# A layer norm's tail tile split ahead of its second pair, and the scaling of q spread over four gates

## The reference, cut to what matters

```python
# attention with a linear kernel, 8 batches, 8 heads, 576 tokens, head size 64
q_s = exp(q - max(q, -1));  q_s = q_s / (sum(q_s, -1) + 1e-9)
k_s = exp(k - max(k, 2));   k_s = k_s / (sum(k_s, 2) + 1e-9)
x = q_s @ (k_s^T @ v)                       # heads side by side: (8, 576, 512)

# first feed-forward block
h = gelu(x @ w_in)                          # w_in 512 x 1024
u, v = h[..., :512], h[..., 512:]
v_n = (v - mean(v)) / sqrt(var(v) + 1e-6) * g_ln
v_s = w_sg @ v_n + b_sg                     # over the 576 tokens
x = x + (u * v_s) @ w_out

# second feed-forward block
h = relu(x @ w_in2);  gate = sigmoid(conv3(h))
out = (h * gate) @ w_out2
```

## Time and profile before

| | |
|---|---|
| median of 3 runs | 922.87 us (921.62 to 923.33) |
| the profiled execution's own time | 924.54 us |
| its span in the trace | 922.6 us |
| PE busy | 905.7 us (98%) |
| DVE busy | 644.9 us (70%) |
| ACT busy | 398.5 us (43%) |
| POOL busy | 371.9 us (40%) |
| granted clock of PE | 0.998 |

### The profile page before, as it was taken

The page is one execution under the profiler, slowest core; times in us unless marked ns, Lnnn a source line. Parts: engine busy times, 40 slices in busy tenths (PEclk is TensorE's granted clock), DMA queues, the critical chain, the costliest instruction groups (busy, mean ns, idle before and its releaser), DMA issues.

```text
span 922.6 us, 14586 instructions
## 1 busy us (share of the span) xinstructions
PE 905.7 (98%) x5852; PEld 843.8 (91%) x5852; DVE 644.9 (70%) x952; ACT 398.5 (43%) x593; POOL 371.9 (40%) x232
## 2 busy tenths in 40 slices
PE   6999999999999999999999999999999999999998
PEld 5799899998998999989989999999999999998987
DVE  6787958678588686765874897866665666757550
ACT  6653544445435444444254254533443343434331
POOL 5773565354472663544514133332232313232320
PEclk9999999999999999999999999999999999999999
DMA  8726674663746546535320302020202020200001
GB/s 294 224 74 230 190 167 154 182 196 123 183 146 175 128 160 179 148 99 137 142 99 30 126 1 87 3 85 23 75 24 86 21 77 23 75 23 24 23 29 52
DMA packets 60034, 99.55 MB, mean 108 GB/s; under 512 B 6720, under 2 KB 25408, under 8 KB 58304
## 3 DMA queue, kind: packets, MB, share of 16 engines
q1 hardware_dynamic: 55360, 89.20, 32.8%
q10 hardware_dynamic: 4608, 9.44, 2.7%
HBM read 78.46 MB, written 19.11 MB: 106 GB/s over the span
## 4 chain that ended last, share of the span: by engine, by line
PE 79%; DVE 6%; POOL 6%; issue 4%; DMA 3%; ACT 2%; SPq 0%; POOLq 0%; DVEq 0%
PE psum L542 45%; PE psum L534 29%; DMA split_arena<-q_rec_dram 2%; DVE plain_arena L1486 2%; PE psum L619 2%; POOL plain_arena L1804 1%; POOL plain_arena L1854 1%; DVE plain_arena L1455 1%; PE psum L655 1%; PE psum L705 1%; POOL split_arena L1848 1%; POOL plain_arena L1811 1%; DMA plain_arena<-in_q_first 1%; PE psum L580 1%; POOL plain_arena L1793 1%
## 5 line engine op out<-in xcount | busy, mean ns | idle before, releaser
L542 PE MATMUL psum<-split_arena 128*128 128x288 f32 x4032 | 558.6, 297 | 1.4 <-DVE split_arena L1518 0.6
L542 PEld LDWEIGHTS psum<-split_arena 128*128 128x128 f32 x4032 | 544.8, 189 | 8.4 <-DVE split_arena L1518 1.9
L534 PE MATMUL psum<-split_arena 128*128 128x512 f32 x1248 | 296.4, 391 | 0.2 <-DVE split_arena L1441 0.2
L534 PEld LDWEIGHTS psum<-split_arena 128*128 128x128 f32 x1248 | 229.9, 188 | 49.3 <-DVE plain_arena L1532 4.3
L1932 POOL TENSOR_TENSOR plain_arena<-plain_arena 128x576 f32<-128x576 f32 x64 | 107.8, 1684 | 277.8 <-ACT plain_arena L1070 277.8
L1577 DVE SCALAR_TENSOR_TENSOR plain_arena<-plain_arena 128x576 f32<-128x576 f32 x64 | 96.2, 1503 | 2.3
L1572 DVE TENSOR_SCALAR plain_arena<-plain_arena 128x576 f32<-128x576 f32 x64 | 36.0, 563 | 87.2 <-ACT plain_arena L1064 87.2
L1064 ACT ACTIVATE plain_arena<-psum 128x576 f32<-128x576 f32 x64 | 41.6, 650 | 105.3 <-PE psum L542 73.9
L1854 POOL TENSOR_TENSOR plain_arena<-plain_arena 128x576 f32<-128x576 f32 x32 | 52.7, 1648 | 62.0 <-DVE plain_arena L1511 62.0
L1843 POOL TENSOR_TENSOR plain_arena<-plain_arena 128x2 f32<-128x2 f32 (+1 forms) x24 | 19.8, 827 | 119.4 <-DVE plain_arena L1472 119.4
L1070 ACT ACTIVATE plain_arena<-plain_arena 128x576 f32<-128x576 f32 x64 | 43.7, 682 | 42.6 <-DVE split_arena L1738 39.5
(11 more groups left out here) (107 smaller groups left out, 831.0 us busy)
## 6 DMA issues: line engine op xcount, KB each, us to landing
x_dram<-plain_arena ACTq DMA_DIRECT2D x32, 288.0 KB, 2.1
plain_arena<-x_dram SPq DMA_DIRECT2D x8, 1152.0 KB, 6.2
out_rows<-plain_arena SPq DMA_DIRECT2D x36, 256.0 KB, 2.0
plain_arena<-in_kT SPq DMA_DIRECT2D x7, 1152.0 KB, 5.4
plain_arena<-in_k SPq DMA_DIRECT2D x7, 1024.0 KB, 5.8
plain_arena<-in_v SPq DMA_DIRECT2D x28, 256.0 KB, 3.9
plain_arena<-in_q_heads SPq DMA_DIRECT2D x6, 1152.0 KB, 8.3
split_arena<-q_max_dram SPq DMA_DIRECT2D x12, 576.0 KB, 10.4
```

The lines of the kernel that those rows point to most:

```text
L534: mm = e.matmul(out, stat[s], mov[m], start=first and n == 0, stop=last and n == 2, skip_group_check=True)
L542: mm = e.matmul(out[:, h, 0:NH], stat[s], mov[m][:, h * NH:(h + 1) * NH], start=first and n == 0, stop=last and n == 2, skip_group_check=True)
```

## The change: what it does

In bodies 1 to 7, POOL makes the inverse deviation of the tail before the first `lo_vn`, and the tail's `lo_vn` before that of pair 1. ACT makes the tail's high half directly behind that of pair 1, both behind `gelu_u(m, 0)`. `move_tail` waits for two of the three low halves, and the third and fourth tile of `sg_unit(m, 0)` for all three.

In bodies 1 to 6, each of the four gates is followed by one tile of q on POOL, ACT and DVE, where the first two gates were followed by two tiles each. The last `hi_q_rows` stands behind `hi_g(m, 3)`, and the last `lo_q_rows` behind `lo_g(m, 3)`.

```diff
@@ SP, move_tail @@
-                e.wait_ge(vn_lo, (b + 1) * NU)
+                e.wait_ge(vn_lo, b * NU + (NU if b == 0 else 2))
@@ PE, sg_unit @@
-                        e.wait_ge(vn_lo, b * NU + j // 2 + 1)
+                        e.wait_ge(vn_lo, b * NU + (1 if j < 2 else 2 if b == 0 else NU))
@@ ACT, body @@
-                    if not start and f == (0 if a is not None else 1):
+                    if not start and f == 0:
                         hi_vn(m, 1)
-                    if not start and f == (1 if a is not None else 2):
                         hi_vn(m, 2)
...
-                    elif a is not None and f in (1, 2):
-                        hi_q_rows(a, 2 * f - 2)
-                        hi_q_rows(a, 2 * f - 1)
+                    elif a is not None and f > 0:
+                        hi_q_rows(a, f - 1)
                     if a is not None and f == FT - 1:
                         hi_kv(a)
...
                     hi_g(m, f)
+                    if not start and a is not None and f == FT - 1:
+                        hi_q_rows(a, f)
@@ DVE, body @@
-                        if f in (1, 2) and a is not None:
-                            lo_q_rows(a, 2 * f - 2)
-                            lo_q_rows(a, 2 * f - 1)
+                        if f > 0 and a is not None:
+                            lo_q_rows(a, f - 1)
...
                 lo_g(m, FT - 1)
+                if a is not None and not start:
+                    lo_q_rows(a, DT - 1)
@@ POOL, body @@
                     inverse_deviation(m, 0)
                     inverse_deviation(m, 1)
+                    inverse_deviation(m, 2)
                     lo_vn(m, 0)
-                    inverse_deviation(m, 2)
+                    lo_vn(m, 2)
                     lo_vn(m, 1)
-                    lo_vn(m, 2)
                 for f in range(FT):
                     gate(m, f)
-                    if not start and a is not None and f < 2:
-                        scale_q_rows(a, 2 * f)
-                        scale_q_rows(a, 2 * f + 1)
+                    if not start and a is not None:
+                        scale_q_rows(a, f)
```

## The result

| | before | after |
|---|---|---|
| median of the runs | 922.83 us (921.62 to 923.33) | 936.62 us (935.77 to 936.96) |
| the profiled execution's own time | 924.54 | 936.58 |
| its span | 922.6 | 934.6 |
| PE busy | 905.7 | 909.7 |

The ratio is 1.0152, 95% interval 1.0139 to 1.0165: slower by 13.8 us, where 4.1 were forecast. The time lies outside the range. The direction was right. The profiled executions lie 12.04 apart, less than the medians, since the one of the kernel before was 1.7 above its median.

What follows compares the result with a forecast made beforehand. With PE 98% busy, the chain started by max_q on DVE was taken to set the length of a body. Terms +3.79 - 0.38 - 0.43 + 1.1 = +4.08 on 922.87 gave 927.0 us, range 923.7 to 929.2.

Steps and rivals of the forecast that it cites:

- `max_q` later, bodies 1 to 5: DVE, bodies 1 to 5: the new q order starts max_q later behind sg_unit and lengthens the bodies, +3.79 us in sum.
- `gelu_u(1)`, body 7: ACT, body 7: gelu_u(1) waits for the tail's normalisation, so PE waits before u_unit(3), +1.1 us.
- `gelu_u(1)`, bodies 2 to 6: ACT, bodies 2 to 6: two kv_piece stand before u_unit(3), so there is room and no cost.
- `gelu_u(1)`, body 1: ACT, body 1: the later gelu_u(1) may lose a few tenths, not counted in the sum.
- body 6: Body 6, without max_q: lo_q(3) hides in DVE's wait for PE, and the wait for lo_g(2) goes, -0.38 us.
- the wait for the moved tail, body 1: PE, body 1: an earlier move_tail brings 0 to 0.86 us; half was taken, -0.43.
- `max_q` sets the body: DVE, bodies with max_q: it starts a chain without slack, so any delay of it lengthens the body by as much.
- the rival "faster": max_q is not the chain; only the removed waits for lo_g (1.9) and the tail (0.86) count: 920.1 us, chance 0.08.
- The price on ACT: Layer norm, body 7: POOL's lo_vn holds the port against DVE's normalise of the tail, delaying gelu_u(1): PE waits +1.1 us.
- the rival "lock goes to DVE": Layer norm, body 7: DVE's normalise wins the port, so the 1.1 falls away: 925.9 us, chance 0.23.
- a rival for bodies 1 to 5 at 0.07: Load of the next k waits for lo_q(3) and overlaps x stores, about 1 us a body: 932 us, chance 0.07.
- The tail's move: SP: move_tail is issued earlier; nothing gained in bodies 2 to 7, -0.43 us in body 1.

Runs made afterwards that it cites:

- Experiment 6: The kernel before with the q part of the change alone, and the last lo_q_rows of bodies 1 to 5 moved behind the two max_q on DVE: 932.56 us.
- kernel 3: The kernel after with gelu_u(m, 1) placed ahead of both hi_vn on ACT in bodies 1 to 7: 929.01 us.
- kernel 5: The kernel after with the tail's inverse deviation on POOL back behind the first lo_vn: 930.19 us.
- Experiment 4: The kernel after with the q tiles in pairs behind the first two gates in body 6 alone: 932.67 us.
- experiment 1: The kernel before with the layer norm part of the change alone, q tiles in pairs as before: 929.36 us.
- experiment 2: The kernel before with the q part of the change alone, layer norm as before: 928.6 us.
- experiment 10: The kernel after with gelu_u(1) ahead of both hi_vn, body 6's q in pairs, max_q behind the first affine, next k loaded behind two x stores: 920.15 us.
- kernel 9: Kernel of experiment 6 with the load of the next k, in bodies 1 to 4, behind the first two of the body's four x stores: 927.16 us.
- kernel 11: The kernel before with the load of the next k, in bodies 1 to 4, moved behind the body's first add_x, over the x stores: 937.54 us.

## Why the prediction was wrong, step by step

In the profiled executions, forecast against measured:

| step | forecast | measured |
|---|---|---|
| `max_q` later, bodies 1 to 5 | +3.79 | +2.32 |
| `gelu_u(1)`, body 7 | +1.1 | +2.1 |
| `gelu_u(1)`, bodies 2 to 6 | 0 | +2.51 |
| `gelu_u(1)`, body 1 | "tenths" | +1.18 |
| body 6 | -0.38 | +2.43 |
| slow matmuls, body 7 | 0 | +1.5 |
| the wait for the moved tail, body 1 | -0.43 | -0.20 |
| start | 0 | +0.16 |
| sum | +4.08 | +12.0 |

- **`max_q` sets the body: right for these two kernels**, and the rival "faster" is out. The offset was put at 20.5 to 20.8 and is 20.3 to 20.5. No wait for `lo_g`, and one of 0.5 to 0.6 for `lo_x`, stand where they were said to. The step was sized too high because locks were added up one after the other; in the kernel after DVE waits 2.04 for `hi_g` in a steady pattern and each gate but the first takes 1.88. The old order's bodies 4 and 5 were taken as body 2 (19.84) and had 19.93 and 19.51, which would have made the step 0.24 larger; the new offset was 1.71 too high over the five bodies. The mechanism has two more conditions. Experiment 6 took `max_q` back to 19.7 and got slower, by the load of k, which I had named only as a rival. And in its body 5, without that load, 0.77 less to `max_q` gave only 0.26: DVE's work ahead of the first `add_x` bounds the body as well.
- **The price on ACT: the failed step.** "DVE's `normalise` of the tail ... finds the port taken" is right, and the rival "lock goes to DVE" is out. But the working let pair 1's `normalise` through before it, and it is held too, 3.13 us in body 2. With it went the sentence on bodies 2 to 6, "and there is room", whose slack I hadn't read (rows below, ACT and PE in body 2 of the kernel before: it ends at 179.79, 0.8 ahead of PE's `u_unit(3)`). It is used up and 0.5 more. Experiments 3 and 5 show it from both ends, by moving the consumer and by moving POOL's instruction. All that hangs on it, the slow matmuls included, is 7.3 us of 12, where I had 1.1.

```profile
179.16 0.63 ACT L994 ACTIVATE plain_arena<-psum 128x576 f32<-128x576 f32 x1
...
180.57 6.62 PE L542 MATMUL psum<-split_arena 128*128 128x288 f32 x48
```

- **Body 6: a missed term with a wrong sign.** "There `lo_q(3)` hides in the time that DVE waits for PE" looked at DVE alone. SP waits for the same instruction, with four bulk loads behind it. I had the mechanism as a rival for bodies 1 to 5 at 0.07 and didn't carry it to body 6. Experiment 4 takes it away: 932.67. The -0.38 itself came as forecast; the missed term is 2.81.
- **The tail's move: no gain shown.** PE's wait shrank by 0.2, within the 0 to 0.86 given, but not for the reason given, by luck: the issue came 0.94 earlier, the landing 1.2 later. With the change's layer norm alone (experiment 1) the tail took 7.2 us to land and PE waited 1.34 for it.
- **The slow matmuls** were in no case of mine. They add to the misses; they don't explain them, and by the mean granted clocks they differ between executions of one kernel (last section).
- **The rest**, 13.8 by the medians against 12.04 by the profiles, is the 1.7 by which the profiled execution of the kernel before lies above its median.

The rule of the Trainium skill on which the prediction leaned (SBUF — State Buffer, "Who interferes with whom") agrees with the traces read here: of a DVE `normalise` or `lo_...` step and a POOL step that meet, one waits the other out in full, 2.38 us in the longest `lo_vn`. What failed was the bookkeeping of who waits.

## What to carry to other kernels

When a step is moved later, list every queue that waits for its semaphore, SP's loads above all, and ask which transfers its release will now lie over. A consumer that is placed behind two producers inherits the locks of both: read its slack from the trace in each body, not just in the one where it is already visible. A spread of work that loses can win once the chain that it delays is taken out of its way: the same q tiles cost 5.1 us in one order (experiment 2) and belong to the fastest kernel in another (experiment 10).

## What the runs showed that I had not expected

- A waiting `normalise` on DVE was not served between two of POOL's instructions that follow without a gap: 3.13 us (3.12 to 3.14 in the seven bodies), from within the inverse deviation (0.81) to behind `lo_vn` (2.38), in place of 0.55.
- A store of 288 KB that lands in 2.1 us alone took a median of 5.5, and up to 6.7, with bulk loads of another queue over it. Moving one such load in each of four bodies cost 14.9 us in all (937.54 against 922.62).
- The granted clock fell to 0.50 behind some gaps of PE and not behind others of the same length. It fell behind 1.93 us in body 7 of the kernel after, 2.21 in body 6 of kernel 9 (6 matmuls in 2.89 us where 1.82 is usual), 2.16 in body 6 of kernel 6, and 2.75 and 2.81 in kernel 11. It didn't behind 2.36 in body 6 of the kernel after, 1.95 in kernels 1 and 4, 2.06 in kernel 5, 2.18 in kernel 3, 2.19 in kernel 2 and in body 4 of kernel 6, nor 2.26 and 2.34 in kernel 11. It seems to differ between executions of one kernel as well. A fall of some 3 us to 0.50 takes about 0.002 off the mean; the profile of the kernel before (0.998) has one at 14 to 18 us, ahead of the bodies. The mean granted clocks of kernel 2's six executions are 1.0 three times (925.93, 928.48, 927.28 us), 0.998 once (929.37) and 0.996 twice (928.72, 929.17), and in kernel 11 the slowest execution (940.49) has the lowest, 0.991. Where it fell in the runs without a profile isn't known. What decides it stays open; which kernel has the slow matmuls can't be told from one profile each.
